# Order of the first hidden pair, and of three copies on ACT, in a retention and MLP kernel on one core

## The reference

```
x  = retention(q, k, v)                        # state = gamma*state + k v^T ; y = scale * q state
u  = x + ((x^T @ U) @ V)^T                     # U: 768 x 32, V: 32 x 768
x2 = u + relu(u @ w_ch1) @ w_ch2               # 512 -> 2048 -> 512
h  = relu(x2 @ w_in)                           # 512 -> 1024, halves: u', v
v_n = (v - mean) / sqrt(var + 1e-6)            # over the 512 channels
v_s = w_spatial @ v_n + b_spatial              # over the tokens
out = (u' * v_s) @ w_out
```

## Time and profile before

| | |
|---|---|
| three timed runs | 474.47, 475.24, 475.42 us, median 475.24 |
| profiled execution | 473.94 us, span 471.9 us |
| TensorE busy | 462.0 us, 98% of the span |
| weight loads busy (beside TensorE) | 411.5 us, 87% |
| VectorE busy | 339.2 us, 72% |
| ACT busy | 251.4 us, 53% |
| GpSimd busy | 48.2 us, 10% |
| granted TensorE clock, mean | 0.999 of full speed |
| the chain that ended last | TensorE 91%, VectorE 5%, ACT 2%, DMA 2% |

### The profile page before, as it was taken

One profiled execution on the slowest core, in us unless ns is written; L12 is line 12 of the kernel. 1 busy time (PEld: TensorE's weight loads), 2 busy tenths in 40 slices (PEclk: granted clock), 3 DMA queues, 4 the chain that ended last, 5 costly groups with the idle time before them and its releaser, 6 DMA issues.

```text
span 471.9 us, 8650 instructions
## 1 busy us (share of the span) xinstructions
PE 462.0 (98%) x3140; PEld 411.5 (87%) x3140; DVE 339.2 (72%) x755; ACT 251.4 (53%) x589; POOL 48.2 (10%) x52
## 2 busy tenths in 40 slices
PE   8899998999999999999999999999999999999997
PEld 5788897988999999988888999988888689999997
DVE  4788978887789987874855976774813997794430
ACT  1666755555667655833464655733432855454312
POOL 2178970000000000000100000000100001000000
PEclk9999999999999999999999999999999999999999
DMA  8989801344432343202220343202105002011003
GB/s 282 405 289 315 303 2 45 112 158 133 135 123 91 100 139 121 91 11 78 90 90 1 107 138 115 91 7 84 44 1 200 1 0 92 0 66 69 0 1 135
DMA packets 20361, 50.31 MB, mean 107 GB/s; under 512 B 1504, under 2 KB 3168, under 8 KB 19168
## 3 DMA queue, kind: packets, MB, share of 16 engines
q1 hardware_dynamic: 19904, 49.24, 30.4%
q10 hardware_dynamic: 416, 0.53, 0.3%
HBM read 46.61 MB, written 3.15 MB: 105 GB/s over the span
## 4 chain that ended last, share of the span: by engine, by line
PE 91%; DVE 5%; ACT 2%; DMA 2%; issue 1%; DVEq 0%; ACTq 0%
PE bank L1413 9%; PE bank L1411 9%; PE bank L1414 9%; PE bank L1394 8%; PE bank L1392 8%; PE bank L1395 8%; PE bank L1532 5%; PE bank L1261 3%; PE bank L1513 3%; PE bank L1516 3%; PE bank L1515 3%; PE bank L1451 2%; PE bank L1453 2%; PE bank L1452 2%; PE bank L1306 2%; PE bank L1300 2%
## 5 line engine op out<-in xcount | busy, mean ns | idle before, releaser
L1392 PE MATMUL bank<-bh,w1c 128*128 128x256 f32 x336 | 94.6, 282 | 1.9 <-DVE hl L985 1.9
L1395 PE MATMUL bank<-bh,w1c 128*128 128x256 f32 x336 | 94.7, 282 | 0.0
L1394 PE MATMUL bank<-bl,w1c 128*128 128x256 f32 x336 | 94.6, 282 | 0.0
L1413 PE MATMUL bank<-hl,w2h 128*128 128x512 f32 x192 | 75.9, 395 | 0.0
L1411 PE MATMUL bank<-hh,w2h 128*128 128x512 f32 x192 | 75.8, 395 | 0.0
L1414 PE MATMUL bank<-hh,w2l 128*128 128x512 f32 x192 | 74.7, 389 | 0.0
L1392 PEld LDWEIGHTS bank<-bh,w1c 128*128 128x128 f32 x336 | 63.5, 189 | 8.7 <-issue 2.1
L977 DVE TENSOR_TENSOR c<-bank,p 128x256 f32<-128x256 f32 x72 | 30.5, 424 | 52.6 <-PE bank L1395 31.4
L1394 PEld LDWEIGHTS bank<-bl,w1c 128*128 128x128 f32 x336 | 63.4, 189 | 5.5
L1395 PEld LDWEIGHTS bank<-bh,w1c 128*128 128x128 f32 x336 | 63.4, 189 | 0.0
L614 ACT ACTIVATE p<-bank 128x256 f32<-128x256 f32 x72 | 27.5, 381 | 48.2 <-PE bank L1395 47.1
(11 more groups left out here) (142 smaller groups left out, 933.2 us busy)
## 6 DMA issues: line engine op xcount, KB each, us to landing
w1raw<-w SPq DMA_DIRECT2D x24, 512.0 KB, 5.0
w2raw<-w SPq DMA_DIRECT2D x24, 512.0 KB, 4.1
att<-attn SPq DMA_DIRECT2D x7, 1152.0 KB, 7.8
att<-attn SPq DMA_DIRECT2D x10, 384.0 KB, 5.4
out_T<-stage SPq DMA_DIRECT2D x7, 384.0 KB, 2.4
wsp_raw<-w_sp SPq DMA_DIRECT2D x1, 2304.0 KB, 8.3
winraw<-w_in SPq DMA_DIRECT2D x4, 512.0 KB, 5.0
tab<-decay SPq DMA_DIRECT2D x7, 258.0 KB, 4.8
```

The source lines that it names most:

```text
L1392: mm(o, w1c[k][:, 0, q, s], bh[:, q, c, :], start=(opens and c == 0), stop=False, skip_group_check=True)
L1394: mm(o, w1c[k][:, 0, q, s], bl[:, q, c, :], start=False, stop=False, skip_group_check=True)
L1395: m = mm(o, w1c[k][:, 1, q, s], bh[:, q, c, :], start=False, stop=(c == 1), skip_group_check=True)
L1413: mm(ch_ps[c][:, :], w2h[h][:, s], hl[k][:, h, :], start=False, stop=False, skip_group_check=True)
```

## The change

No instruction is added or taken away on any engine; the order changes, and with it the counts that three waits ask for.

In the first pair, the relu and the rest that free the bank (s = 2) move ahead of those with 512 columns (s = 1), and `HID_FIRST` gives the new positions in hid_hi. `product(1, 1)` waits for two rests of hl instead of three, `ch2(0, ...)` for all three in both halves. The roundings and rests of w1 operands 4 to 6 of pair 1 move from the end of pair 0 into pair 1, behind its first copy (ACT) and its first sum (VectorE). `p_rest` of the last item moves there too, `p_round` goes behind two roundings of w1, `up` moves from behind `product(1, 0)` to behind `product(1, 4)`, `u_add` to the end of pair 1. The first ch2 group of pair 0 comes after `product(1, 2)` instead of after `product(1, 1)`, and the rest of them one step later, too.

On ACT, `relu_in(2, 0)` and `relu_in(2, 1)` move ahead of the first two roundings of w_spatial, and `sp_copy(a, 0)` for a = 1 and 3 ahead of the last rounding of the product before, `round_g(a - 1, 3)`.

```
@@ ACT, pairs @@
                     elif n == 1:
+                        round_w1(n, range(4, NQ))
...
+                    round_w1(n + 1, range(2, 4))
+                    if n == 0:
                         p_round(NI - 1)
-                    round_w1(n + 1, range(2, 4))
...
+                    if n == 0:
+                        relu_hid(n, 2)
                     relu_hid(n, 1)
                     if n:
                         round_w2(n, 0)
-                    relu_hid(n, 2)
-                    if n == 0:
-                        round_w1(n + 1, range(4, 7))
+                        relu_hid(n, 2)
@@ ACT, third stage @@
+            relu_in(NT - 1, range(0, 2))
             round_wsp(0)
             round_wsp(1)
-            relu_in(NT - 1, range(0, 2))
@@ ACT, fourth stage @@
             for a in range(NA):
-                sp_copy(a, 0)
+                if a % 2 == 0:
+                    sp_copy(a, 0)
...
                 round_g(a, 2)
                 if a == 0:
                     round_wout(range(2, CT))
+                if a % 2 == 0:
+                    sp_copy(a + 1, 0)
                 round_g(a, 3)
@@ VectorE @@
+        HID_FIRST = (1, 3, 2)
-                dve.wait_ge(hid_hi, 3 * n + s + 1)
+                dve.wait_ge(hid_hi, 3 * n + s + 1 if n else HID_FIRST[s])
...
                     sum_c(n, 0)
+                    if n == 1:
+                        rest_w1(n, range(4, NQ))
+                        p_rest(NI - 1)
...
                     if n == 0:
                         sum_c(n, 1)
                         sum_c(n, 2)
-                        p_rest(NI - 1)
+                        rest_hid(n, 0)
                     weight_sums(n + 1, range(3, 4))
...
-                    rest_hid(n, 0)
                     if n:
+                        rest_hid(n, 0)
                         rest_w1(n + 1, range(6, 7))
-                    else:
-                        rest_w1(n + 1, range(2, 4))
-                    rest_hid(n, 1)
-                    if n:
+                        rest_hid(n, 1)
                         rest_w2(n, 0)
                     rest_hid(n, 2)
                     if n == 0:
-                        rest_w1(n + 1, range(4, 7))
+                        rest_w1(n + 1, range(2, 3))
+                        rest_hid(n, 1)
+                        rest_w1(n + 1, range(3, 4))
+                    if n == 1:
                         u_add(NI - 1)
@@ TensorE @@
                 if n and q == 1:
-                    pe.wait_ge(hid_lo, 3 * n)
+                    pe.wait_ge(hid_lo, 3 * n if n > 1 else 2)
...
-                    pe.wait_ge(hid_lo, 3 * n + 2 + h)
+                    pe.wait_ge(hid_lo, 3 * n + 2 + h if n else 3)
...
                     product(n, 0)
                     if n == 1:
-                        up(NI - 1)
-                    for q in range(1, 7):
+                        product(n, 1)
+                    for q in range(2 if n == 1 else 1, 7):
                         product(n, q)
-                        ch2(n - 1, q - 1)
+                        if n == 1 and q == 4:
+                            up(NI - 1)
+                        ch2(n - 1, q - (2 if n == 1 else 1))
+                    if n == 1:
+                        ch2(n - 1, 5)
```

More of the change, by code:

```diff
@@ L696, in _ @@
                         xn_copy(NI - 1, 1)
-                    elif n > 1:
+                    elif n == 1:
+                        round_w1(n, range(4, NQ))
+                    else:
                         round_w2(n - 1, 1)
```

## The result

The changed kernel takes 469.88 us (median of 4 runs, 469.66 to 470.04) against 475.33 us for the kernel before (4 runs, 474.47 to 475.61): ratio 0.9888, 95% interval 0.9871 to 0.9905. The profiled execution took 469.91 us for a span of 467.9, so its span is 4.0 us shorter than the one of before. In the later series three single executions (506, 567 and 1598 us) are left out of every median and count.

What follows compares the result with a forecast made beforehand. TensorE, busy 98% of the span, was taken as the bound, with three waits behind the opening. Gains 1.5 + 1.0 + 0.8 = 3.3 us, taken off the median 475.24, gave 471.9 us; range 471.0 to 472.8, stretched to 470.3 and 473.6.

Steps and rivals of the forecast that it cites:

- The three places: TensorE's waits in pair 1, last token group and batch 0's second spatial product; removing them gains 3.3 us.
- Place one: Pairs 0 and 1: product (1,1) waits for two hl rests instead of three; gain 1.5 us, bounds 1.0 to 1.6.
- The slacks of 0.1 and 0.2 us: Pair 1: margins by which p5 for (1,5) and the second sum for (1,6) are ready before TensorE needs them.
- rival (b): Pair 1: VectorE operations at 0.42 instead of 0.34 overrun the slacks; total gain 2.4, 472.8 us; chance 0.09.
- Place two: Last token group: relus emptying the banks run before two w_sp roundings; gain 1.0 us, bounds nothing to 1.1.
- The roundings' delay: Last token group: the two w_sp roundings move 2.3 us later, with 4 us of cover before VectorE reads them.
- Place three: Second spatial product of batch 0: p1s copied before the gate's rounding; gain 0.95, of which 0.8 us kept.
- The charge of 0.1 to 0.2 for p16s: Second spatial product of batch 0, step five: p16s copied slightly late, costing 0.1 to 0.2 us.
- Rival (a): Spatial product: VectorE does not follow, TensorE waits about 1.0 for p16s; gain 2.5 less the rest, 472.8 us; chance 0.10.
- Batch 1: The same copy exchange in batch 1: copy starts at 442.90 either way; gain nothing, 0.1 us slack, bound 0.3.
- Rival (c): Pair 1: ACT and VectorE alternate in lockstep, a rest costing 0.86 instead of 0.34; slower, 476.5 us; chance 0.04.
- Rival (d): Edits do not take hold: second hl rest's relu or p1s copy still waits for something else; 475 us; chance 0.05.

Runs made afterwards that it cites:

- E1: The kernel before, unchanged, measured again: 474.81 us (12 executions), ratio to before 1.0012.
- E5: The changed kernel, unchanged, measured again: 470.13 us (6 executions), ratio to before 0.9925.
- E3: The kernel before with only the two relus moved ahead of the first two roundings of w_sp: 472.15 us, ratio 0.9965.
- E4: The kernel before with only the p1s copies moved ahead of the gate's rounding, in both batches: 473.12 us, ratio 0.9986.
- E7: The kernel before with 12 matmuls that nobody reads put into its pair 1 standstill: 473.58 us, ratio 0.9985.
- E10: The changed kernel, product 1 of pair 1 held for the fourth w1 rest, V's two small operations ahead of that rest: 473.21 us, ratio 0.9982.

## Why the prediction was wrong

The three places were read rightly: they gave 3.6 us (1.57, 1.07 and 0.95), where 3.3 were forecast. The step that failed is in the sum: the 3.3 us, worked out on one profiled execution, were "taken off" the median of 475.24, 1.3 us above that execution, so that the 1.3 us stayed in the forecast of 471.9. They did not stay: after the change the median (469.88) and the profiled execution (469.91) are the same. What the runs show in their place is the fall of the clock behind the standstill of pair 1, 1.5 us in E1's profile, which the profiled execution of before did not have and its timed runs very likely had. They list no clocks, so this last link is argued and not shown, but three of the four (475.24, 475.42, 475.61) lie above every full-clock execution of before in the later series (at most 474.58), and inside the group at 0.996 or below. The change took away the standstill and the fall with it.

So the forecast missed by 2.0 us: 1.3 by this term, 0.3 by the three places, 0.3 by an opening that was shorter in this execution, 0.1 by the last part. The prediction knew of the 1.3 us and let them into the range, but not into the sum or a rival. Its lower end of 470.3 is the profiled execution less the upper bounds of all three places (473.94 less 1.6, 1.1 and 0.95); it had no room for the last two terms, 0.4 us, and the result lies that much below it.

The size of the measured gain is partly luck of the draw. In the later series 24 of 63 executions of before have the fall, so three or more of four come about one time in six; with 17 executions of before beside it the changed kernel is 4.0 us faster (E5), not 5.45.

Point by point:
- Place one, forecast 1.5: in the two profiles of the changed kernel 1.6 by the distance from the product with U. The forecast chain, shifted by the 0.32 us of the opening, gives product 1 at 73.92 and pair 2 at 84.18; they were at 73.93 and 84.16. The slacks of 0.1 and 0.2 us held, so rival (b) fell. This place carried the missing term: a fall costs 1.5 us in E1's profile (17.57 against 16.05) and 1.2 to 2.1 between the medians of a kernel's two groups, in 4 executions of 10.
- Place two, forecast 1.0: 1.07, alone (E3) as together. The roundings' delay was covered, as written.
- Place three, forecast 0.8: 0.95, alone 0.86 (E4). The charge of 0.1 to 0.2 for p16s came true (0.12). What the sum left out is the restart of 0.08 that went with the wait (405.23 to 405.48 is 0.25 for a step of 0.17), and 0.05 in the spatial products that came with place two (39.31 in E3). Rival (a) fell, VectorE followed. Its sum of 398.65 started at 395.66, 3.0 us earlier with TensorE; the 0.4 us by which it comes late in both profiles stay unexplained, and cost nothing.
- Batch 1, forecast nothing: the last part, to the end, is 58.69 to 58.79 us in every profile. Nothing.
- Rival (c), lockstep of ACT and VectorE: VectorE stayed at 0.33 a step. Rival (d): all three edits took hold.

The profiled execution was forecast at 470.6 and took 469.9: 0.3 from the opening, 0.3 from the three places together, 0.1 from the last part.

What stays open: the time of the opening varies from one execution to the next (the product with U starts between 69.05 and 70.30 us in the profiles here), which is as large as the effects of places two and three; and why the fall comes in some executions and not in others with the same standstill.

## What to carry to other kernels

Read the granted clock of several executions, not of one profile: when the median of the timed runs lies well above the profiled execution (here 1.3 us), something that comes and goes may be missing from the profile, and a change may remove it. A standstill of TensorE should be priced twice, once at its length and once at what the clock loses behind it; if the wait can't be removed, a few matmuls that nobody reads in it are worth trying (E7: 1.6 us of them, and the median fell to that of the full-clock executions). For the waits themselves the chain of releases, row by row, was good to 0.2 us a place (1.57 for 1.5, 1.07 for 1.0, 0.95 for 0.8).

## What the runs showed that was not expected

With a standstill of 1.9 us, in a TensorE that is otherwise busy 98% of the time, 40 of 97 executions had a mean clock of 0.996 or below, with one of 1.2 or 1.5 us none of 12, and with one of 2.25 us 8 of 12. In the two such executions that were profiled the clock stood at half for 3.4 us. The fall begins 0.4 to 0.6 us after TensorE has taken up work again (76.10 after 75.67 in E1, 76.55 after 75.98 in E10), not during the standstill, so the row of the wait itself looks the same with and without it.
